# First routing of a capacity-limited expert layer: one threshold search with 16 candidates per step, weight casts on ScalarE, rows gathered ahead of most weights

## What is computed

```python
logits = x @ w_gate                      # 3072 x 8
order = np.argsort(-logits.flatten())
for idx in order:                        # greedy, best logit first
    tok, e = idx // 8, idx % 8
    if assigned[tok] >= 0 or counts[e] >= 384: continue
    assigned[tok] = e; counts[e] += 1
out[mask_e] = np.maximum(x[mask_e] @ w1[e], 0) @ w2[e]   # per expert
h = out @ w_in; solu = h * softmax(h)
result = ((solu - mean) / sqrt(var + 1e-6) * g_ln) @ w_out
```

## Time and profile before

| | |
|---|---|
| median of three runs | 820.72 us |
| the three runs | 817.78, 821.66, 820.72 us |
| the profiled execution's own time | 817.24 us |
| its span, first to last instruction | 815.5 us |
| mean granted TensorE clock | 0.942 |
| TensorE, VectorE, ScalarE, GpSimd busy | 703.3, 577.9, 343.4, 332.5 us |

### The profile page before, as it was taken

One profiled execution on the slowest core, in us unless ns is written; L12 is line 12 of the kernel. 1 busy time (PEld: TensorE's weight loads), 2 busy tenths in 40 slices (PEclk: granted clock), 3 DMA queues, 4 the chain that ended last, 5 costly groups with the idle time before them and its releaser, 6 DMA issues.

```text
span 815.5 us, 17673 instructions
## 1 busy us (share of the span) xinstructions
PE 703.3 (86%) x6837; PEld 611.8 (75%) x6838; DVE 577.9 (71%) x2165; ACT 343.4 (42%) x551; POOL 332.5 (41%) x243
## 2 busy tenths in 40 slices
PE   4679983116998999999999999999999999999993
PEld 3457762015987898979898888989798989898882
DVE  3458888877878868886978788778868886741140
ACT  3458771012225713651473256235613741563170
POOL 2000019967417613751574067127614740572001
PEclk9899996557998999999999999999999999999997
DMA  8979974134013202310331133023203311330000
GB/s 235 289 250 296 321 244 134 52 104 142 1 52 117 78 27 90 117 52 27 117 117 53 52 104 103 27 65 117 78 27 91 125 70 52 104 104 27 1 14 39
DMA packets 24385, 83.88 MB, mean 103 GB/s; under 512 B 4032, under 2 KB 4096, under 8 KB 24320
## 3 DMA queue, kind: packets, MB, share of 16 engines
q0 software_dynamic: 14208, 50.34, 19.1%
q1 hardware_dynamic: 10112, 32.72, 13.1%
HBM read 70.46 MB, written 12.58 MB: 102 GB/s over the span
## 4 chain that ended last, share of the span: by engine, by line
PE 61%; DVE 10%; POOL 9%; DMA 8%; issue 7%; ACT 3%; SPq 1%; POOLq 0%; DVEq 0%; ACTq 0%
PE bank L529 17%; PE bank L530 15%; PE bank L531 15%; POOL wl L1311 6%; DMA raw<-w,w_idx 5%; PE bank L462 2%; PE banks L444 2%; DMA vr<-v_in 2%; PE bank L419 2%; DVE hits L974 2%; PE bank L429 1%; POOL raw L1305 1%; PE bank L455 1%; DVE z L1103 1%; DVE hot_a L974 1%
## 5 line engine op out<-in xcount | busy, mean ns | idle before, releaser
L1311 POOL TENSOR_TENSOR wl<-raw,wh 128x1024 fp32r<-128x1024 f32 x60 | 146.5, 2443 | 20.9 <-ACT wh L747 19.9
L1305 POOL DMA_INDIRECT raw<-w,w_idx x60 | 65.0, 1084 | 161.4 <-DVE w_idx L1023 123.7
L747 ACT ACTIVATE wh<-raw 128x1024 fp32r<-128x1024 f32 x60 | 63.3, 1056 | 83.0 <-DMA raw<-w,w_idx 82.9
L529 PE MATMUL bank<-xh,wh 128*128 128x384 f32 x256 | 91.2, 356 | 3.6 <-POOL wl L1311 3.4
L529 PE MATMUL bank<-hh,wh 128*128 128x384 f32 x256 | 90.1, 352 | 0.0
L530 PE MATMUL bank<-xl,wh 128*128 128x384 f32 x256 | 87.0, 340 | 0.0
L531 PE MATMUL bank<-xh,wl 128*128 128x384 f32 x256 | 87.0, 340 | 0.0
L531 PE MATMUL bank<-hh,wl 128*128 128x384 f32 x256 | 86.0, 336 | 0.0
L530 PE MATMUL bank<-hl,wh 128*128 128x384 f32 x256 | 85.9, 336 | 0.0
L529 PE MATMUL bank<-wout_h,uh 128*128 128x512 f32 x192 | 79.1, 412 | 0.2
L529 PE MATMUL bank<-win_h,yh 128*128 128x512 f32 x192 | 77.3, 403 | 0.0
(11 more groups left out here) (180 smaller groups left out, 1660.5 us busy)
## 6 DMA issues: line engine op xcount, KB each, us to landing
unit<-qk_in SPq DMA_DIRECT2D x24, 768.0 KB, 9.1
vr<-v_in SPq DMA_DIRECT2D x48, 130.0 KB
x_rows<-x_sb SPq DMA_DIRECT2D x24, 256.0 KB, 6.1
raw<-w_in POOLq DMA_DIRECT2D x4, 512.0 KB, 4.6
raw<-w_out POOLq DMA_DIRECT2D x4, 512.0 KB, 3.9
vr<-v_mem SPq DMA_DIRECT2D x32, 32.5 KB
raw<-w,w_idx POOLq DMA_INDIRECT x60, 4.4
gath<-x_rows,ids POOLq DMA_INDIRECT x24, 3.5
```

Source lines behind the costliest of these rows:

```text
L529: nc.tensor.matmul(bank, stat_h, mov_h, start=first, stop=False)
L747: nc.scalar.activation(wh[:, c % WCH, :], stage(s, c), ACT.Copy).then_inc(w_hi, 1)
L1305: gp.indirect_dma_start(stage(s, c), None, table, bass.IndirectOffsetOnAxis(ap=w_idx[:, c % WCH:c % WCH + 1], axis=0))\
L1311: gp.tensor_tensor(wl[:, c % WCH, :], stage(s, c), wh[:, c % WCH, :].bitcast(F32), ALU.subtract)\
```

## The change

1. **First routing.** For f = 0 the votes aren't transposed. VectorE compares the best value of each token with 16 candidates (15 steps and the present one) in two halves, each 128x192, and writes ones and zeros in bf16. TensorE counts them for all experts in 24 small products (16 columns held, 8 moving). VectorE tests which counts reach 384, and one more product spreads the result. The maximum over experts is the next digit: one threshold for all experts, four bits per level, eight levels. The scratch tiles lie in `hot_b` and PSUM.
2. **flips** is written after the first routing's ids, ahead of `best_open(1)`; `steps` is written where it was.
3. **ROUNDS_FIRST**: two rounds ahead (three before), one per h group as before, seven in the y groups.
4. **Preparation**: SP loads the eight pieces to buffers of their own once attention's last product is done; ScalarE scales and casts; GpSimd only subtracts, from when Vm is written. TensorE waits for it at the first z group, ScalarE after the first rows.
5. **GpSimd's order at the start**: weight pieces 0 and 1; ids; row gathers; low part 0; pieces 2 and 3; low part 1; pieces 4 to 7.
6. VectorE's semaphore counting is simplified, and the counts of f start at 1.

```diff
-ROUNDS_FIRST = rounds_of([[0, 0, 0]], [[2], [2], [2], [3], [3], [3], [3], [3]], [[], []], [[6], [3], [0, 5], [2, 7]])
+ROUNDS_FIRST = rounds_of([[0, 0]], [[2], [2], [2], [3], [3], [3], [3], [3]], [[], []], [[1, 5], [1, 5], [1, 5], [3]])
...
+        at_least, is_best = hot_b[:, :, 0:WAYS], hot_b[:, :, WAYS:WAYS + E]
+        steps = hot_b[:, 0:LEVELS, 32:32 + 2 * WAYS].bitcast(I32)
+        prep_at = [prep_first[:, n, :] for n in range(6)] + [prep_rest[:, n, :] for n in range(2)]
...
+        cand_16, following_16 = WIDE[:, 400:400 + WAYS].bitcast(I32), WIDE[:, 416:416 + WAYS].bitcast(I32)
...
+            sp.wait_ge(pv_ps, NT)
+            for n in range(8):
+                if n == 6:
+                    sp.wait_ge(logits_ps, 1)
+                sp.dma_start(prep_at[n], w_in[n, :, :] if n < 4 else w_out[n - 4, :, :]).then_inc(prep_loaded[n], 16)
...
+            def level(n):
+                for j in range(2):
+                    pe.wait_ge(compared, 2 * n + j + 1)
+                    for t in range(TG * j, TG * j + TG):
+                        mm = nc.tensor.matmul(TOT[0:WAYS, 0:E], at_least[:, t, :], is_best[:, t, :],
+                                              start=(t == 0), stop=(t == NT - 1))
+                mm.then_inc(level_ps, 1)
+                pe.wait_ge(reached_ready, n + 1)
+                nc.tensor.matmul(TOT[:, 8:8 + E], ones_b[0:WAYS, :], reached[:, :], start=True, stop=True)\
+                  .then_inc(digit_ps, 1)
...
+                if s == 0 and g == 0:
+                    pe.wait_ge(prep_lo, 8)
...
-            best_T(0)
-            for j in range(SEARCH):
-                total(0, j)
-            thresholds(0)
+            for n in range(LEVELS):
+                level(n)
             ranks(0)
             token_ids(0)
             best_T(1)
             total(1, 0)
             rows_T(0, [0])
             total(1, 1)
-
-            pe.wait_ge(prep_lo, 8)
             rows_T(0, [1, 2])
-            total(1, 2)
             keep_warm(3)
             expert(0, first=True)
             for s in range(1, E - 1):
...
+                    if g < 2 and first:
+                        weight_hi(s, 2 + g)
...
+            for n in range(8):
+                act.wait_ge(prep_loaded[n], 16)
+                if n >= 4:
+                    for a in range(2):
+                        k, piece = 2 * (n - 4) + a, prep_at[n][:, 512 * a:512 * a + 512]
+                        nc.scalar.activation(piece, piece, ACT.Copy, scale=gain[:, k:k + 1]).then_inc(prep_scaled, 1)
+                    act.wait_ge(prep_scaled, 2 * (n - 3))
+                nc.scalar.activation(prep_high(n), prep_at[n], ACT.Copy).then_inc(prep_hi, 1)
             weight_hi(0, 0)
             weight_hi(0, 1)
-            weight_hi(0, 2)
-            weight_hi(0, 3)
             row_high(0)
+            act.wait_ge(prep_lo, 8)
...
+            nc.vector.memset(reached[:, :], 16.0)
+            for k, n, turn in ((0, 7, -1), (7, 15, -1 << 31)):
+                nc.vector.tensor_scalar(steps[:, 0, k:n], ways[:, k:n], LEVEL_SHIFT[0], turn,
+                                        ALU.logical_shift_left, ALU.bitwise_xor)
+            nc.vector.memset(steps[:, 0, WAYS - 1:WAYS], 0)
+            for n in range(1, LEVELS):
+                turn = shifted_int(SIXTEEN, LEVEL_SHIFT[n - 1] - SIXTEEN_SHIFT) if n > 1 else -1 << 31
+                nc.vector.tensor_scalar(steps[:, n, :], ways[:, :], LEVEL_SHIFT[n], turn,
                                         ALU.logical_shift_left, ALU.bitwise_xor)
...
+            def first_search():
+
+                done(nc.vector.tensor_reduce(best[:, :, :], over_e(M[:, :, :, :]), AX.X, ALU.max))
+                done(nc.vector.tensor_tensor(is_best.rearrange("p (j t) e -> p j e t", j=2), M[:, :, :, :],
+                                             best[:, :, :].unsqueeze(2).to_broadcast([P, 2, E, TG]), ALU.is_equal))
+                for n in range(LEVELS):
+                    tried = cand_16 if n else steps[:, 0, :]
+                    for j in range(2):
+                        nc.vector.tensor_tensor(at_least[:, TG * j:TG * j + TG, :],
+                                                best[:, j, :].unsqueeze(2).to_broadcast([P, TG, WAYS]),
+                                                tried.bitcast(F32).unsqueeze(1).to_broadcast([P, TG, WAYS]),
+                                                ALU.is_ge).then_inc(compared, 1)
+                    if n == 0:
+                        done(nc.vector.tensor_scalar(mask[:, :, :, :], is_best.rearrange("p (j t) e -> p j e t", j=2),
+                                                     -2.0 * NEG, NEG, ALU.mult, ALU.add))
+                        nc.vector.tensor_tensor(Vm[:, :, :, :], M[:, :, :, :], mask[:, :, :, :], ALU.min)\
+                          .then_inc(vm_ready, 1)
+                    elif n < LEVELS - 1:
+                        done(nc.vector.tensor_tensor(following_16, steps[:, n + 1, :],
+                                                     cand_16[:, WAYS - 1:WAYS].to_broadcast([P, WAYS]), ALU.bitwise_xor))
+                    else:
+                        done(nc.vector.tensor_scalar(following_16[:, 0:1], cand_16[:, WAYS - 1:WAYS],
+                                                     shifted_int(SIXTEEN, -SIXTEEN_SHIFT), None, ALU.bitwise_xor))
+                    ve.wait_ge(level_ps, n + 1)
+                    rows = WAYS - 1 if n < LEVELS - 1 else WAYS
+                    nc.vector.tensor_scalar(reached[0:rows, :], TOT[0:rows, 0:E], float(CAP), None, ALU.is_ge)\
+                      .then_inc(reached_ready, 1)
+                    ve.wait_ge(digit_ps, n + 1)
+                    done(nc.vector.tensor_reduce(digit[:, :], TOT[:, 8:8 + E], AX.X, ALU.max))
+                    if n == 0:
+                        done(nc.vector.tensor_scalar(below[:, :], digit[:, :], 24.0, -1.0, ALU.is_lt, ALU.mult))
+                        done(nc.vector.scalar_tensor_tensor(out=following_16, in0=below[:, :].to_broadcast([P, WAYS]), scalar=1,
+                                                            in1=steps[:, 1, :], op0=ALU.logical_shift_right,
+                                                            op1=ALU.bitwise_xor))
+                    if n < LEVELS - 1:
+                        left = LEVEL_SHIFT[n] - SIXTEEN_SHIFT
+                        done(nc.vector.scalar_tensor_tensor(
+                            out=cand_16, in0=digit[:, :].bitcast(I32).to_broadcast([P, WAYS]), scalar=abs(left),
+                            in1=following_16, op0=ALU.logical_shift_left if left >= 0 else ALU.logical_shift_right,
+                            op1=ALU.bitwise_xor))
...
+                if f == 0:
+                    top = digit
+                else:
+                    top = t_max
+                    ve.wait_ge(thresholds_ps, f)
+                    done(nc.vector.tensor_reduce(t_max[:, :], T, AX.X, ALU.max))
...
+                if f == 0:
+                    done(nc.vector.tensor_scalar(digit[:, :], digit[:, :], 15.0, None, ALU.add))
+                    done(nc.vector.scalar_tensor_tensor(out=t_max[:, :].bitcast(I32), in0=digit[:, :].bitcast(I32),
+                                                        scalar=SIXTEEN_SHIFT, in1=following_16[:, 0:1],
+                                                        op0=ALU.logical_shift_right, op1=ALU.bitwise_xor))
...
-            best_open(0)
-            begin_search(0)
-            search(0, enumerate(range(SEARCH)))
-            end_search(0)
+
+            first_search()
             choose(0)
             place(0)
             write_ids(0)
+            for j in range(SEARCH):
+                nc.vector.tensor_scalar(flips[:, j, :], digits[:, :], ROUND_SHIFT[j + 1] if j + 1 < SEARCH else 0,
+                                        shifted_int(FOUR, ROUND_SHIFT[j] - FOUR_SHIFT) if j else 0,
+                                        ALU.logical_shift_left, ALU.bitwise_xor)
             best_open(1)
             begin_search(1)
...
+            gp.wait_ge(vm_ready, 1)
...
+                gp.tensor_tensor(prep_low(n), prep_at[n], prep_high(n).bitcast(F32), ALU.subtract).then_inc(prep_lo, 1)
...
-                    for c in range(6):
-                        fetch_weights(s, c)
-                    weight_lo(s, 0)
-                else:
-                    fetch_weights(s, 0)
-                    fetch_weights(s, 1)
...
+                    weight_lo(s, 0)
+                    for c in range(2, 4):
+                        fetch_weights(s, c)
                     weight_lo(s, 1)
-                    fetch_weights(s, 6)
-                    fetch_weights(s, 7)
+                    for c in range(4, 8):
+                        fetch_weights(s, c)
                 else:
```

More of the change, by code:

```diff
@@ L62 @@
 FOUR, FOUR_SHIFT = 0x40800000, 21
+LEVELS, WAYS = 8, 16
+LEVEL_SHIFT = [28 - 4 * n for n in range(LEVELS)]
+SIXTEEN, SIXTEEN_SHIFT = 0x41800000, 19
 def shifted_int(x, left):
```

91 lines of the change are left out of this document (38 added, 53 removed).

## The result

The changed kernel took **797.37 us** (median of 4 runs, 794.11 to 799.38) beside 821.19 us for the kernel before (4 runs, 817.78 to 822.01). The ratio is 0.9717, 95% interval [0.9679, 0.9755]: about 23 us less, between 20 and 26. The forecast was 800.0, 20 to 21 less, with a range of 793 to 808. The profiled execution took 797.4 us; its span is 795.6, 19.9 less than before.

A forecast was written before the change was run, and what follows sets the result against it. TensorE was taken to idle before the first expert, behind search, choose, place, gather. Terms: -21.5 + 1.3 + 0.4 = -19.8, making the profiled 817.24 797.4; with the runs' average 2.8 higher, forecast 800.0 us, range 793 to 808.

The forecast's parts named there:

- The level: First routing's search: one level of comparing, counting, testing, spreading and maximum takes 2.26 us, with bounds 2.0 to 7.2.
- Rivals 2: First search: each handoff over TensorE costs 0.5 more, a level 3.3; result 806; chance 0.12 together with Rival 5.
- 4: First search: the 24 small products of a level don't overlap, a level takes 7.2; result 840; chance 0.02.
- VectorE against GpSimd: Beside GpSimd's subtractions comparisons run free; following_16 waits 1.6 us, e_hot until the eighth ends; w_idx starts at 152.35.
- rival 3: Blocked VectorE instruction gets no turn between subtractions and waits for all eight; 16.5 worse, result 816.5; chance 0.05.
- Rows and weights: Gathers for the first expert: rows stand 1.0 behind ids, 4.7 before; weights cost nothing, last margin 1 us.
- Rival 5: GpSimd is still in preparation or weights when ids is ready; result 803 to 808; chance 0.12 together with Rivals 2.
- Flips: The 17 flips, now between ids and best_open, take 1.56 us on the way to the first expert product.
- The y groups: First expert: TensorE waits 1.9 in the first y group, less 0.6 for diag; second expert starts 1.3 later.
- Rival 1: No wait in y group 0 (-1.3) and clock stays up at the second expert (-3); result 796; chance 0.13.
- The clock at the first product: First expert: TensorE's higher clock level may come up to 3 us later than its first product; +0.4.
- From the second expert on: Clock at the second expert's start expected the same as before, the other experts unchanged: no difference.

The follow-up runs named there:

- e_psum: Changed kernel with level 1's steps kept in PSUM, so following_16 no longer has two SBUF operands: 797.87 us.
- e_psum_defer: As e_psum, with the last two of GpSimd's eight subtractions put behind the sixth and seventh weight subtractions: 796.85 us.
- e_rounds: Changed kernel with the first expert's seven y rounds at k = [5], [1,5], [1,5], [1,5], the first one later: 797.22 us.
- e_all_2: Second run of e_all's kernel, in another group beside the changed kernel: 792.47 us.
- e_all: Changed kernel with four edits: later y rounds, flips ahead of the logits, level 1's steps in PSUM, two subtractions put off: 796.80 us.
- e_best: e_all's four edits plus the second expert's row low parts moved earlier on VectorE in the first expert: 794.56 us.
- after_again: The changed kernel run again, unchanged, in a further group: 798.85 us.
- e_before_order: Kernel before with only the first expert's fetches reordered, row gathers right after weight pieces 0 and 1: 816.94 us.
- e_oldsearch: Changed kernel with the old 17-round first search put back and flips ahead of the logits, all else as changed: 811.92 us.

## Why the prediction was right

Its account of the way to the first expert product holds step by step, and the stretches behind it only in sum; each distance below is from the start of the copy of M at 129.87 in the prediction's sum.

| step | forecast | measured |
|---|---|---|
| M to first comparison | 1.28 | 1.95 |
| M to the comparison of level 1 | 5.63 | 5.99 |
| one level | 2.26 | 2.11 |
| eight subtractions | 19.2 | 18.48 |
| M to w_idx | 22.48 | 21.90 |
| w_idx to ids | 9.74 | 9.67 |
| ids to first row gather | 1.0 | 0.95 |
| ids to first expert product | 11.0 | 10.30 |
| M to first expert product | 43.2 | 41.87 |
| wait in first y group | 1.9 | 1.74 |

*The level* was built from pieces, and the piece it hung on, 24 products like token_ids', was right in kind: 0.75 together, of which 0.54 stands behind the comparisons (0.56 forecast). A level is 0.15 shorter since each piece is a little below its price, the lone product that spreads the result most (0.18 instead of 0.24). Rivals 2 and 4 fall with it.

*VectorE against GpSimd.* Of all steps this one was least certain, since no row showed VectorE between two subtractions in a row. It gets its turn when the running one ends (following_16, e_hot), so rival 3 falls. The comparisons, best in SBUF and candidates in PSUM, take 0.62 a pair beside the subtractions and 0.63 before them, so the levels run free. And the claim that w_idx hangs on the last subtraction, however fast the search, is what e_psum showed. That w_idx was early by only 0.6 hides larger terms: the subtractions took 0.7 less (2.31 each, not 2.40), but began 0.6 later, since is_best took 1.01 instead of the 0.36 that I had priced it at; the sum had their end 0.3 later than its own 132.6 + 19.2, and w_idx starts 0.07 behind that end instead of 0.25. One row was misread without harm: L962's 1.008 was beside a cast, not a subtraction.

*Rows and weights.* Rival 5 falls: GpSimd had waited 7 us when ids came. The weights cost nothing, which e_psum_defer shows with less cover.

*Flips.* 1.36 instead of 1.56 (the row's own pitch gives 1.51), and worth 0.4 rather than their length when put elsewhere. The forecast chain went from the flips over the second round's counting to the transpositions; with the flips gone it goes over the landing of the rows. The term had the right sign, and its cover was misjudged.

*The y groups.* The wait is where it was forecast and of its size, but the term around it, 1.9 - 0.6 = +1.3, was too small. In the first profile, where the clock stood at 1.00, it is +1.9: the y groups take 2.26 more than before (19.71 against 17.45), 1.74 of it the wait, and from there to the second expert only 0.33 is saved. Two steps failed here. The 0.6 for a wait for diag had no row: TensorE shows no idle time before the product at 230.87. And the clock: I let it fall only at the second expert, and behind this wait it fell in two of the three profiles of the changed kernel, where H0->H1 grew by 3.9 and 4.1, 1.6 of it from this fall and 0.3 to 0.6 from the clock at the first product. Rival 1 wanted this wait gone; it isn't in the changed kernel, and e_rounds shows what that would have given.

*The clock at the first product.* +0.4 was forecast, for a higher level that comes up to 3 us later, which no row showed. The three profiles of the changed kernel have 0, 0.85 and 1.58 us at the lower level in the first expert and h groups longer by 0, 0.3 and 0.6. Of all profiles of kernels with M->H0 between 39 and 42, only the first one and e_all_2 were spared; e_all and e_best lost 1.7 us. So the term was right in size, and what it costs differs from one execution to the next.

*From the second expert on.* I forecast no difference, and it is -1.2, the sum of three larger ones: -1.1 to the third expert's first product, +2.8 over the next five experts, -2.8 from the last expert's first product on. The first is the clock behind the gap ahead of the second expert (6.8 us at the lower level before, 3.4 here); but after_again had 6.8 again and the same step as before or longer (77.56 against 77.41), so it is scatter and no part of rival 1. The second comes from a quick profile before: 378.1 us, where all other profiles have 378.7 to 380.9. The third is real and was overlooked. Timelines of TensorE, in the last expert, before and then changed:

```profile
736.29 0.98 PE L558 MATMUL banks<-ident,z 128*128 128x128 f32 x7 [1.99 <-ACT z L768]
```

```profile
717.72 0.98 PE L603 MATMUL banks<-ident,z 128*128 128x128 f32 x7 [0.60 <-ACT z L810]
```

This wait is 1.99 before and 2.20 in e_before_order, and behind it the clock stands at 0.50 for 3.4 us. In the twelve other kernels and repeats the wait is 0.5 to 1.7 and the clock stays up, and from the last expert's first product to the end they take 103.4 to 104.5 us instead of 106.3. So 2 to 3 us come from a stretch that the forecast took to be unchanged. All twelve have the moved preparation, seven rounds in the first y groups and VectorE's simplified counting, which e_before_order lacks; how any of these reaches the last expert no run shows.

The sum was -19.8 and the span's difference -19.9, and that closeness is luck: M->H0 gained 1.3 more than the forecast's 21.5, the y groups and the clock lost 1.9 instead of 1.3 + 0.4, the rest gave 1.2, and M came 2.2 later, which is mostly scatter. From M to the end the three profiles of the changed kernel are 22.0, 19.7 and 21.3 shorter than the one of the kernel before. The medians say 23 to 24; the last 2 or 3 of these us no pair of profiles shows, though the one profile before was among its kernel's quicker executions (817.24 beside a median of 821.19).

## What to carry to other kernels

When a chain of small dependent steps over two engines bounds a stretch, count the round trips: 8 levels of 2.1 us with 16 candidates beat 17 rounds of 2.1 with 3, since here a step with 16 candidates took as long as one with 3. A background stream on GpSimd wasn't free for VectorE, though nothing waited for its results there: look at which operands of the critical instructions lie in SBUF, and which is the last to meet the stream, since speed gained ahead of that one is lost there. Before an instruction is moved forward, see who waits for those that it is put before.

## What the hardware showed that I had not expected

A TensorE wait of only 1.7 us in full work was followed by the lower clock level in six of eight profiles and not in the other two, at a cost of 1.65 us in the pair above, about that of the wait itself. An earlier start of the first expert can be paid back in part to the clock: 4.0 us at the lower level in e_all, none in e_all_2, with the same edits. is_best, 128x192 with an output in another order and in bf16, took 1.01 us with GpSimd idle, where the contiguous f32 form of the same comparison took 0.36 (e_oldsearch; also the earlier trace rows); that is the missing 0.65 ahead of the first comparison, and whether order or type makes it wasn't tried. And the copy of M, after 130 us of attention that no edit touched, scattered by 4 us between profiles, a sixth of the whole gain: single spans of two kernels say nothing about anything smaller.
